# Retention, mixture of experts and MLP in one kernel: token parts of 128, 512 and 512, and a second layer that leaves PSUM after every stage

## The reference

```python
# 1 retention, per head (8 heads of 64): linear attention with decay
scores = scale * q @ k.T
ret    = scores * gamma ** (i - j)        # for j <= i, else 0
x      = ret @ v                          # -> (1152, 512)
# 2 mixture of 4 experts, every token goes through all four
for e in range(4):
    h = maximum(x @ w1[e], 0)             # 512 -> 1024
    out += p[:, e:e+1] * (h @ w2[e])      # 1024 -> 512
# 3 MLP
h = out @ w_in                            # 512 -> 2048
g = h * tanh(softplus(h))                 # mish
y = g @ w_out                             # 2048 -> 512
```

## Time and profile before

| | |
|---|---|
| time, median of 3 | 631.87 us (630.59 to 632.71) |
| profiled execution | 630.54 us, its span 628.8 us |
| PE busy | 620.6 us, 99% of the span, 3764 matmuls |
| PEld busy | 553.7 us, 88% |
| DVE busy | 243.5 us, 39% |
| ACT busy | 238.0 us, 38% |
| POOL busy | 284.4 us, 45% |
| HBM traffic | 79 GB/s over the span |

### The profile page before, as it was taken

The page is one execution under the profiler, slowest core; times in us unless marked ns, Lnnn a source line. Parts: engine busy times, 40 slices in busy tenths (PEclk is TensorE's granted clock), DMA queues, the critical chain, the costliest instruction groups (busy, mean ns, idle before and its releaser), DMA issues.

```text
span 628.8 us, 9476 instructions
## 1 busy us (share of the span) xinstructions
PE 620.6 (99%) x3764; PEld 553.7 (88%) x3765; DVE 243.5 (39%) x388; ACT 238.0 (38%) x459; POOL 284.4 (45%) x239
## 2 busy tenths in 40 slices
PE   8999999999999999999999999999999999999997
PEld 5788899998999999899999899989979999999996
DVE  5756743333143333143323143335564333314324
ACT  3555433332223432223432223435544455334432
POOL 4759535543435542535543535532553544443300
PEclk9999999999999999999999999999999999999999
DMA  8954312222112322102321202321100232201002
GB/s 275 339 177 158 111 34 68 100 88 64 51 35 67 101 84 67 51 34 67 101 84 56 62 35 67 101 67 47 55 34 34 68 116 85 68 0 52 1 0 100
DMA packets 25146, 50.41 MB, mean 80 GB/s; under 512 B 2896, under 2 KB 3216, under 8 KB 25104
## 3 DMA queue, kind: packets, MB, share of 16 engines
q1 hardware_dynamic: 24816, 49.66, 24.2%
q10 hardware_dynamic: 288, 0.17, 0.1%
HBM read 47.45 MB, written 2.36 MB: 79 GB/s over the span
## 4 chain that ended last, share of the span: by engine, by line
PE 95%; DVE 3%; ACT 1%; issue 0%; POOL 0%; DVEq 0%; ACTq 0%; POOLq 0%
PE bank L480 30%; PE bank L482 30%; PE bank L481 30%; PE bank L434 2%; PE bank L474 2%; DVE xt L896 1%; PE bank L612 1%; PE bank L605 1%; PE bank L438 1%; DVE acc_sb L866 0%; DVE acc_sb L870 0%; ACT h_hi L708 0%; DVE h_lo L826 0%; DVE acc_sb L975 0%; ACT h_act L691 0%
## 5 line engine op out<-in xcount | busy, mean ns | idle before, releaser
L381 POOL TENSOR_TENSOR w_lo<-w_raw,w_hi 128x512 fp32r<-128x512 f32 x96 | 128.8, 1356 | 151.0 <-ACT w_hi L354 151.0
L482 PE MATMUL bank<-w_hi,h_lo 128*128 128x512 f32 x432 | 169.9, 393 | 0.0
L481 PE MATMUL bank<-w_lo,h_hi 128*128 128x512 f32 x432 | 169.5, 392 | 0.0
L480 PE MATMUL bank<-w_hi,h_hi 128*128 128x512 f32 x432 | 169.0, 391 | 0.0
L376 POOL TENSOR_TENSOR ws<-ws_f,ws 128x1024 fp32r<-128x1024 f32 x24 | 57.9, 2412 | 150.4 <-ACT ws L350 150.4
L853 DVE TENSOR_TENSOR h_act<-part,bank 128x384 f32<-128x384 f32 x96 | 52.8, 550 | 179.4 <-PE bank L482 179.4
L482 PEld LDWEIGHTS bank<-w_hi,h_lo 128*128 128x128 f32 x432 | 81.0, 188 | 17.5
L481 PEld LDWEIGHTS bank<-w_lo,h_hi 128*128 128x128 f32 x432 | 81.0, 188 | 9.8
L480 PEld LDWEIGHTS bank<-w_hi,h_hi 128*128 128x128 f32 x432 | 81.1, 188 | 9.6
L703 ACT ACTIVATE h_hi<-h_act 128x384 fp32r<-128x384 f32 x64 | 33.6, 526 | 104.8 <-DVE h_act L853 104.8
L713 ACT ACTIVATE part<-bank 128x384 f32<-128x384 f32 x72 | 35.2, 489 | 82.9 <-PE bank L482 82.2
(11 more groups left out here) (87 smaller groups left out, 916.0 us busy)
## 6 DMA issues: line engine op xcount, KB each, us to landing
w_raw<-in_weights SPq DMA_DIRECT2D x144, 256.0 KB, 2.7
qkv<-in_chunks SPq DMA_DIRECT2D x18, 512.0 KB, 4.9
out<-acc_sb SPq DMA_DIRECT2D x6, 256.0 KB, 2.0
out<-acc_sb SPq DMA_DIRECT2D x1, 768.0 KB, 5.3
consts<-in_consts ACTq DMA_DIRECT2D x1, 146.0 KB, 3.8
ident<-in_consts SPq DMA_DIRECT2D x1, 64.0 KB, 4.0
consts<-in_consts SPq DMA_DIRECT2D x1, 34.0 KB, 4.0
p_nat<-in_probs ACTq DMA_DIRECT2D x1, 18.0 KB, 3.9
```

Source lines behind the costliest of these rows:

```text
L381: pool.tensor_tensor(w_lo[:, layer, x], w_raw[:, r % RAW], w_hi[:, layer, x].bitcast(F32), ALU.subtract).then_inc(s_wl, 1)
L480: pe.matmul(out, w[0], x[0], start=first, stop=False, **more)
L481: pe.matmul(out, w[0], x[1], start=False, stop=False, **more)
L482: return pe.matmul(out, w[1], x[0], start=False, stop=last, **more)
```

## The change

- Tokens are in parts of 128 (`xa`), 512 and 512 (`xb`). The products of the two large parts have 512 columns. The plain part has 128 columns, and both hidden tiles of a stage write one bank (4 or 5).
- All stages are alike now: 4 per expert, 24 in all, each with 7 products for two hidden tiles and one plain piece of 2 tiles (`first_tile`, 24 matmuls of 128 columns). The first stage of the experts and of the MLP (`FRESH`) have two such pieces ahead of their products and hardly any second layer between them.
- The second layer is computed per stage and token tile: 6 matmuls of 512 columns into one of four rotating banks, 9 tiles per stage, and VectorE adds each to `acc_sb` (216 times in place of 54).
- Retention has no layer work in its turns, and the weights come later.
- At the switch all 9 token tiles are transposed first, between the second layer's pieces of the stage before, and the MLP's first stage follows.
- Weights: rings of 3 stages, 6 raw buffers in place of 8.

```diff
-TC = 384
-PH = TOKENS // TC
-TT = TC // P
+NB = 512
+BT = NB // P
-RAW = 8
+RAW = 6
+RING = 6
-AFTER_SCORES = {8: (0, 1), 9: (1, 1), 10: (2, 1), ...
-AFTER_OUTPUT = {7: (0, 0), 8: (1, 0), 9: (2, 0), 10: (3, 0), 11: (4, 0)}
-STAGES = 6
+STAGES = UNITS // 2
+FRESH = (0, MOE_STAGES)
+ACCS = 4
...
+            def first_tile(s):
+                pe.wait_ge(s_wl, JOB["w1", s, 1] + 1)
...
+                for i in range(2):
+                    for k in range(KT):
+                        at = slice(P * k, P * (k + 1))
+                        mm = three(first_bank(s)[:, i], (w_hi[:, 0, ring(s, i), at], w_lo[:, 0, ring(s, i), at]),
+                                   (xa_hi[:, k], xa_lo[:, k]), k == 0, k == KT - 1)
+                mm.then_inc(s_a1, 1)
...
-                    mm = three(banks[BANK_OF[j]][:, 0:TC], w, x, j in OPENS and k == 0, k == KH - 1,
+                    mm = three(banks[BANK_OF[j]][:, :], w, x, j in OPENS and k == 0, k == KH - 1,
...
+            def second(s, t):
+                n = seconds(s, t)
+                pe.wait_ge(s_wl, JOB["w2", s, 1] + 1)
+                if t == 0:
+                    pe.wait_ge(s_al, s + 1)
+                else:
+                    pe.wait_ge(s_hl, ITEMS * s + (C21 if t <= BT else C12) + 1)
+                if n > ACCS:
+                    pe.wait_ge(s_af, n - ACCS)
+                cols = slice(P * t, P * (t + 1))
+                for i in range(2):
+                    mm = three(banks[(n - 1) % ACCS][:, :], (h_hi[:, s % 2, i, cols], h_lo[:, s % 2, i, cols]),
+                               (w_hi[:, 1, ring(s, i)], w_lo[:, 1, ring(s, i)]), i == 0, i == 1)
+                mm.then_inc(s_acc, 1)
...
             for c in range(TURNS):
                 if c < CHUNKS:
                     scores_and_state(c)
-                if c in AFTER_SCORES:
-                    plain_half(*AFTER_SCORES[c])
                 if c == 0:
                     keep_warm(3)
                 if c > 0:
                     output(c - 1)
-                if c in AFTER_OUTPUT:
-                    plain_half(*AFTER_OUTPUT[c])
...
+            for s in range(ALL_STAGES):
                 if s == MOE_STAGES:
+                    for t in range(TPP):
+                        second(s - 1, t)
+                        if t > 0:
+                            turn(t - 1)
+                    turn(TPP - 1)
+                if s in FRESH:
+                    first_tile(s)
+                    first_tile(s + 1)
+                    for j in (P1, P2, P6):
+                        product(s, j)
+                    second(s, 0)
+                    for j in (P7, P5, P4, P3):
+                        product(s, j)
+                else:
+                    ts = tiles_in(s)
                     for j in range(7):
                         product(s, j)
+                        second(s - 1, ts[j])
+                    if s - 1 not in FRESH:
+                        first_tile(s)
+                    for t in ts[7:]:
+                        second(s - 1, t)
+            for t in range(TPP):
+                second(ALL_STAGES - 1, t)
```

More of the change, by code:

```diff
@@ L88, with tiles_in @@
 OPENS = (P1, P2, P5, P4)
[L90 to L118, removed]
+T_ORDER = (1, 2, 0, 3)
+ACCS = 4
+def tiles_in(s):
+    return range(int(s - 1 in FRESH), TPP) if s not in FRESH else ()
 JOBS, IN_TURN, IN_STAGE = [], {}, {}
@@ L405, in _ @@
             load_chunk(1)
-            for c in range(2, 6):
+            for c in range(2, CHUNKS):
                 if c > 2:
@@ new lines, in turn @@
+            def turn(t):
+                if t == 0:
+                    pe.wait_ge(s_id, 16)
+                    pe.wait_ge(s_cc, ITEMS * MOE_STAGES)
+                if t == 2:
+                    pe.wait_ge(s_x2l, 1)
+                if t > 2:
+                    pe.wait_ge(s_x2f, t - 2)
+                pe.wait_ge(s_af, seconds(MOE_STAGES - 1, t))
+                for d in range(KT):
+                    mm = pe.transpose(turn_bank(t)[:, d], acc_sb[:, t, P * d:P * (d + 1)], ident[:, :])
@@ new lines, in add_up @@
+            def add_up(s, t):
+                e, n = s // STAGES, seconds(s, t)
+                dve.wait_ge(s_acc, n)
+                ps, acc = banks[(n - 1) % ACCS][:, :], acc_sb[:, t]
+                if e < MOE_EXPERTS:
+                    p = p_norm[:, t, e:e + 1]
+                if s in FRESH and t == 0:
+                    dve.wait_ge(s_tl, 4 * (e > 0) + 4)
+                if s == 0:
+                    dve.tensor_scalar(acc, ps, p, None, ALU.mult).then_inc(s_af, 1)
+                elif e < MOE_EXPERTS:
+                    dve.scalar_tensor_tensor(acc, ps, p, acc, ALU.mult, ALU.add).then_inc(s_af, 1)
+                elif s == MOE_STAGES:
+                    dve.tensor_copy(acc, ps).then_inc(s_af, 1)
+                else:
+                    dve.tensor_tensor(acc, ps, acc, ALU.add).then_inc(s_af, 1)
@@ L981, in _ @@
-            sum_lo(ALL_STAGES - 1, C12)
-            add_up(EXPERTS - 1, 1)
-            add_up(EXPERTS - 1, 2)
+                else:
+                    ts = tiles_in(s)
+                    add_up(s - 1, ts[0])
+                    add_parts(s, C11)
+                    add_up(s - 1, ts[1])
+                    sum_lo(s, C11)
+                    add_up(s - 1, ts[2])
+                    add_up(s - 1, ts[3])
+                    add_parts(s, C22)
+                    add_up(s - 1, ts[4])
+                    sum_lo(s, C22)
+                    add_parts(s, C21)
+                    add_up(s - 1, ts[5])
+                    sum_lo(s, C21)
+                    add_parts(s, C12)
+                    add_up(s - 1, ts[6])
+                    sum_lo(s, C12)
+                    if s - 1 not in FRESH:
+                        first_tile_lo(s)
+                    for t in ts[7:]:
+                        add_up(s - 1, t)
@@ L985, in _ @@
+            for t in range(TPP):
+                add_up(ALL_STAGES - 1, t)
         @block.gpsimd
@@ L1003, in _ @@
                     job_lo(pool, job)
-            for s in range(1, ALL_STAGES):
+            for s in range(ALL_STAGES):
                 for job in IN_STAGE.get(s, ()):
```

677 lines of the change are left out of this document (265 added, 412 removed).

## The result

| | before | after |
|---|---|---|
| median | 631.63 us | 665.66 us (665.13 to 667.19) |
| ratio | | 1.0543, 95% interval 1.0517 to 1.0568 |
| profiled span | 628.8 us | 663.2 us |

A forecast was written before the change was run, and what follows sets the result against it. TensorE, busy 99% of the span, was taken as the bound. Retention 45, narrow matmuls 63.4, 512-column matmuls 528.3, transposes 4.0, waits 4 + 5 and end 3.4 summed to a 653.1 us span; forecast 654, range 640 to 670.

The forecast's parts named there:

- the cost of the narrow matmuls: Plain pieces: 576 matmuls of 128 columns, each held to 0.11 us by its weight load, 63.4 us in all.
- Rival 1: Plain pieces: loads run further ahead, so 128-column matmuls cost 0.069 us each and the total is 630; chance 0.13.
- rival 3: Plain pieces: narrow fp32r matmuls need more passes, 0.229 us each, 69 us more, total 722; chance 0.05.
- the stage: Expert stages: four stages, one expert, take 98.6 us where an expert took 95.98; a stage lasts 24.6.
- VectorE and the banks cost nothing: Every stage: VectorE has 14 us of work in 24.6, covered by a second-layer tile of 1.4 us between products.
- rival 2: Every stage: VectorE's adding frees product banks late, 10 to 19 us over 24 stages, total 663 to 673; chance 0.13.
- retention: Start of the kernel: TensorE's retention work, without layer work in its turns, ends at 45 us.
- the halves simply stood on top of the turn: Retention before: two layer halves added 2.11 us to a 1.83 us turn and lay in no existing TensorE waits.
- The guard: Retention: its end could slip to 48 us if GpSimd's weight splitting, packed into turns 12 to 18, delays the turns.
- the waits of stages 0 and 1: First stage of the experts: TensorE waits 2.5 to 7 us for token sums and low parts, taken as 4.
- Rival 4: Plain retention turns: the clock falls to the 1.2 GHz level, some 10 us more, total 664; chance 0.04.
- the switch: Switch to the MLP: TensorE waits 3 to 9 us, taken as 5, with transposes staying at 4.0 us.

The follow-up runs named there:

- e2: Changed kernel with the plain piece computed from high parts alone, 8 matmuls per stage in place of 24; one run, 629.9 us.
- e3: Kernel before with its eight plain tiles moved from the retention turns to behind them; 644.78 us, ratio 1.0205.
- e6: Kernel before, plain tiles behind retention, GpSimd's splits inside retention cut to 32 of 512 columns; 637.37 us, ratio 1.0089.
- e1: Changed kernel with the plain piece streaming its 128 columns twice, 256 per matmul, same weight loads; 668.46 us, ratio 1.0588.
- e9: Changed kernel with token parts of 256, 448, 448, second-layer splits ahead of weight-block sums, six first weight blocks' transfers issued earlier; 642.73 us, ratio 1.0181.

## Why the forecast was right, and what it missed

**Right: the cost of the narrow matmuls,** 0.11 forecast and 0.112 measured, on which the sign hung. Rival 1 (0.069) and rival 3 (0.229) are out. The 81 ns of the Trainium skill, "TensorE: Matmul & The Clock Gate", section "Back-to-back issue gap", don't hold for the fp32r matmuls here.

**Right: the stage.** 98.6 us per expert forecast, 98.96 measured. The 0.09 per stage make 2.1 us over 24.

**Right: VectorE and the banks cost nothing** in steady stages; rival 2 is out by the windows and by e2.

**Wrong in its reason, near in its size: retention.** Forecast 45, measured 46.5, 1.5 us. The step that failed is "the halves simply stood on top of the turn ... none of them lay in waits that TensorE had anyway". The plain turn of 1.83 us that it was compared with lies between 13.84 and 19.34, and GpSimd's first split is at 20.79: it has no split in it. The halves hid GpSimd's splits and the VectorE operations that wait beside them. In the kernel before, without the halves, this is 13 us (e3), of which 7.4 are shown to hang on the splits (e6).

In the changed kernel chunk 6 is scaled at 23.71, 0.6 earlier than worked out; the six turns from there to 35.66 take 1.0 more than 1.83 each, while GpSimd's v step waits for the chunks' transfers, and the four to 44.88, with GpSimd's splits in them, 1.9 more. It has 7 jobs in the turns where before had 15, which may be why it pays less; this wasn't tested. The guard that I gave, "if GpSimd's splitting of weights ... delays the turns" up to 48, was the mechanism that occurred. That the profile ends at 46.5 is partly luck: the same code ended at 49.74 in e1 and 48.74 in e2, outside the guard. The lower bound of 43.7 should have been 43.5 (96 x 0.176 is 16.9).

**Mis-sized: the waits of stages 0 and 1.** 4 forecast, 9.8 measured, the largest term of the miss (5.8 us). Their first stretch, 46.48 to 62.00, is 15.5 us for 8.1 of full-rate work (48 x 0.112 + 12 x 0.2293). The forecast weighed the chain of token sums (7.8, and up to 3 more beside GpSimd) against TensorE's 8.0 and took the difference. The chain really ran from 46.65, the last scaling, to 58.7, 12.1 us: the last high part starts 1.0 us late at 48.05, behind `ws` and a weight's high part on ScalarE, the low part takes 1.90 in place of 1.3, the sums 2.18, 2.17 and 1.63.

Rival 4, the fall of the clock, held 0.04 and came true: after turns with TensorE half idle (3.02 busy of 6 us) the granted clock was 0.50 from 46 to 62. Its sign, a PEclk digit below 9 in the first three slices, is in the page (998). Its price of 10 us was too high: at full clock TensorE would still have waited for the sums until 58.7, so that 3.3 us at this product are the most that the clock cost. That 664 lies near the measured 665.7 is chance. The late end of retention is also less of a loss than the table says: stage 2's low part stands at 115.89 here, and at 116.10 in e1, whose retention ended 3.3 us later.

The other 2.4 us are gaps between starts beyond the usual spacing, mainly at two waits, 0.42 (at 71.28) and 1.09, the second behind a low part of 2.01 us beside GpSimd:

```profile
73.99 0.47 PE L457 MATMUL bank<-w_hi,h_hi 128*128 128x512 f32 x1 [1.09 <-DVE h_lo L753]
```

**Mis-sized: the switch,** 5 forecast, 5.9 measured (0.9 us). Its waits in the timeline of PE, with 0.27 more at 468.21, sum to 4.3:

```profile
456.39 0.63 PE L540 MATMUL bank<-ident,acc_sb 128*128 128x128 f32 x4 [0.50 <-DVE acc_sb L779]
...
471.25 0.50 PE L457 MATMUL bank<-xt,ws 128*128 128x512 f32 x1 [1.38 <-DVE h_act L764]
...
477.12 0.47 PE L457 MATMUL bank<-xb_hi,w_hi 128*128 128x512 f32 x1 [1.08 <-DVE h_act L764]
479.77 0.47 PE L457 MATMUL bank<-w_hi,h_hi 128*128 128x512 f32 x1 [1.04 <-POOL ws L359]
```

The last is put down to GpSimd, whose operation ended at 479.12; VectorE's low part (478.33, 1.34 us) ended at 479.67, 0.10 before the start, as it did at the same place in stage 1, so that it is the likelier cause. A wait costs more than its idle time says, since records overlap: counted from start to start, the gaps at these five places and a short one at 474.37 are 5.4 us beyond the usual spacing, and the slower second start behind each makes up the rest of the 5.9. The transposes are as forecast: a second-layer tile with four of them comes every 1.83 us, 1.38 without, and nine times the difference is 4.1.

With 1.5, 2.1, 5.8 and 0.9 the four misses make 10.3 us, against 10.1 between the summed span of 653.1 and the measured 663.2.

## What to carry to other kernels

- Choose parts of tokens so that no fp32r matmul with its own 128 by 128 load has under 256 columns: 128 columns cost 0.112 us, 256 cost 0.12.
- Work that seems to stand on top of a chain can be what keeps two other engines apart. Before taking it out, look at what GpSimd does in the same turn, and at which VectorE operations have both operands in SBUF.
- When the clock falls in a stretch, ask what would bind at full clock there before paying for warmth. Here the operand of the next product was ready 3.3 us before TensorE, and no more than that could be won.
- An end of a chain read from one profile can be off by microseconds: three kernels with the same retention code ended it at 46.48, 48.74 and 49.74.

## What was not expected of the hardware

- The price of a 128-column matmul follows the granted clock: in the stretch at 0.50 they start every 0.21 us, nearly twice the 0.112 of full clock:

```profile
46.75 0.42 PE L458 MATMUL bank<-xa_lo,w_hi 128*128 128x128 f32 x1
46.96 0.41 PE L459 MATMUL bank<-xa_hi,w_lo 128*128 128x128 f32 x1
```

- A VectorE operation of 0.29 to 0.43 us took 1.40 to 4.28 beside unbroken GpSimd operations of 0.7 to 1.3 us (1.40 in the changed kernel, 4.28 in e1 with the same code); those that read a bank kept their 0.40 to 0.68 in the same turns.
- GpSimd is held up as well: an addition of 0.72 to 0.79 us took 1.5 to 1.6 beside VectorE's token sums (e9).
